# A delta-rule attention with two feed-forward layers on one core: products within a chunk over 128 rows beside the Gram products, and tile 1's matrix handed to GpSimd in the middle of VectorE's first inverse

## The reference

```
k_n = k / (norm(k) + 1e-6)
for t in range(S):
    y[t]  = q[t] @ state
    v_old = k_n[t] @ state
    state = state + beta[t] * outer(k_n[t], v[t] - v_old)
```

## Time and profile before

| | us |
|---|---|
| median of 3 runs | 1130.83 (1129.53 to 1133.27) |
| the profiled execution, its own time | 1131.52 |
| span of the profiled execution | 1129.7 |
| TensorE matmuls busy | 1026.9 |
| VectorE busy | 870.2 |
| ScalarE busy | 779.8 |
| GpSimd busy | 227.1 |

### The profile page before, as it was taken

How to read it: one execution, slowest core, us unless ns; L and a number is a source line. 1 busy time by engine, 2 the same in 40 slices (tenths; PEclk the granted TensorE clock), 3 DMA queues, 4 the chain that set the end, 5 groups by cost and what they waited for, 6 DMA issues and landing times.

```text
span 1129.7 us, 24251 instructions
## 1 busy us (share of the span) xinstructions
PE 1026.9 (91%) x10280; PEld 816.6 (72%) x10280; DVE 870.2 (77%) x948; ACT 779.8 (69%) x991; POOL 227.1 (20%) x380
## 2 busy tenths in 40 slices
PE   4488888888778999999999997999999999999997
PEld 3266666666667888777787876778888888888885
DVE  5966666565388888897887868999787878888885
ACT  1133444465598999989989987986776767676764
POOL 5087888880000010010010000000000000000000
PEclk7578999899989999999999999999999999999999
DMA  7823443323443333435234363430100001010000
GB/s 178 237 60 101 115 130 101 84 77 101 118 91 77 80 91 73 111 63 123 56 67 116 60 168 85 121 112 1 57 1 23 32 0 56 0 56 1 29 1 28
DMA packets 35104, 86.99 MB, mean 77 GB/s; under 512 B 4416, under 2 KB 12096, under 8 KB 35008
## 3 DMA queue, kind: packets, MB, share of 16 engines
q1 hardware_dynamic: 27584, 59.13, 17.3%
q0 software_dynamic: 6912, 25.17, 11.7%
q10 hardware_dynamic: 512, 1.31, 0.5%
HBM read 46.27 MB, written 14.16 MB: 53 GB/s over the span
## 4 chain that ended last, share of the span: by engine, by line
PE 34%; DVE 20%; ACT 12%; issue 6%; DMA 1%; ACTq 0%; DVEq 0%; POOLq 0%
PE o_ps L874 6%; PE o_ps L875 6%; PE o_ps L876 6%; PE h_ps L874 6%; PE h_ps L876 6%; PE h_ps L875 6%; DVE val L1098 5%; DVE den L1055 5%; ACT rec L962 4%; DVE pa L1061 3%; ACT rec L970 2%; DVE val L1082 2%; ACT pa L938 2%; DMA val<-pa 1%; DVE den L1089 1%
## 5 line engine op out<-in xcount | busy, mean ns | idle before, releaser
L874 PE MATMUL o_ps<-g_hi,w_hi_early 128*128 128x512 f32 x288 | 115.6, 401 | 20.8 <-DVE g_lo L1104 15.4
L951 ACT ACTIVATE g_hi<-val 128x1024 fp32r<-128x1024 f32 x96 | 102.0, 1062 | 41.8 <-DVE val L1098 36.1
L865 POOL DMA_DIRECT2D val<-pa x48 | 41.4, 862 | 424.5 <-DVE pa L1061 424.5
L874 PE MATMUL o_ps<-g_hi,w_hi_late 128*128 128x512 f32 x288 | 114.1, 396 | 10.4 <-DVE g_lo L1104 9.9
L1098 DVE SCALAR_TENSOR_TENSOR val<-den,val 128x1024 f32<-128x1024 f32 x96 | 117.4, 1222 | 5.0
L1082 DVE TENSOR_TENSOR val<-val,rec 128x1024 f32<-128x1024 f32 x96 | 117.0, 1219 | 5.5 <-DMA val<-pa 5.5
L1104 DVE SCALAR_TENSOR_TENSOR g_lo<-val,g_hi 128x1024 fp32r<-128x1024 f32 x96 | 117.7, 1226 | 2.0 <-ACT g_hi L951 2.0
L875 PE MATMUL o_ps<-g_lo,w_hi_early 128*128 128x512 f32 x288 | 113.9, 396 | 0.0
L876 PE MATMUL o_ps<-g_hi,w_lo_early 128*128 128x512 f32 x288 | 113.5, 394 | 0.0
L874 PE MATMUL h_ps<-x_hi,w_hi_early 128*128 128x512 f32 x288 | 112.3, 390 | 0.7 <-DVE x_lo L1108 0.4
L875 PE MATMUL o_ps<-g_lo,w_hi_late 128*128 128x512 f32 x288 | 112.9, 392 | 0.0
(11 more groups left out here) (114 smaller groups left out, 2175.4 us busy)
## 6 DMA issues: line engine op xcount, KB each, us to landing
val<-pa POOLq DMA_DIRECT2D x48, 512.0 KB, 4.6
w_raw<-w SPq DMA_DIRECT2D x16, 768.0 KB, 5.1
kv_run<-kv_n SPq DMA_DIRECT2D x24, 384.0 KB, 3.8
x_raw<-x_dram SPq DMA_DIRECT2D x12, 768.0 KB, 5.7
kq<-kq_t SPq DMA_DIRECT2D x44, 192.0 KB, 4.0
x_dram<-stage SPq DMA_DIRECT2D x12, 384.0 KB, 4.3
x_dram<-stage SPq DMA_DIRECT2D x6, 768.0 KB, 4.2
out<-stage SPq DMA_DIRECT2D x5, 768.0 KB, 4.1
```

The costliest lines, as they stand in the source:

```text
L874: nc.tensor.matmul(dst, hi, rhs_hi, start=first, stop=False)
L951: act_fn(g_hi[:, n % 2], val[:, n % 2], ACT.Copy, scale=-1.0).then_inc(g_hi_ready, 1)
```

## The change

1. `wide(tau, c)` holds where both steps of a chunk lie beside Gram products: all chunks of tiles 0, 1, 2 and chunks 0 and 1 of tile 3, 28 steps. There `within` takes 4 products over all 128 rows and columns in place of 16 over 32. For that ScalarE spreads `p_mat` into a block-diagonal `p_blk` (four ACTIVATEs a chunk, one for each batch, two in each step, plus four for the first chunk before the steps), and VectorE makes `u_row`, u without its four copies, right after u_blk. TensorE waits for both before the wide products.
2. VectorE stops its inverse of tile 0 after 16 of 31 rounds, does weights(1), the four scale_gram(1) and turn_n(1), then the other 15 rounds. GpSimd's inverse of tile 1 waits for turn_n(1) only.
3. The buffer k_norm is dropped. The keys for the norms go to x_raw (tiles 0 and 2 to 5) and stage (tile 1). Tile 3's keys are loaded after sums(2), and its sums, roots, root_inverse and weights stand later in tile 0. The first load of x for the feed-forward part comes at the end of tile 3's steps in place of tile 2's.

```diff
+def wide(tau, c):
+    return tau < T and len(gram_parts(tau, G2 * c + 1)) > 0
...
-        k_norm = sb("k_norm", [P, CG, D])
+        u_row = sb("u_row", [P, G2, U, D])
+        p_blk = sb("p_blk", [P, 2, HEADS, B, C])
...
             def load_norm(j):
-                if j >= RING:
-                    sp.wait_ge(sumsq_ready, 1 if j == RING else j)
+                if j >= 2:
+                    sp.wait_ge(sumsq_ready, 1 if j == 2 else j)
...
-            load_norm(3)
...
-                if tau and tau + 3 < T:
+                if tau + 3 < T:
                     load_norm(tau + 3)
...
-                if tau == 2:
+                if tau == 3:
+                    sp.wait_ge(sumsq_ready, T)
...
             def within(tau, c, g):
                 q = index(tau, c, g)
                 pe.wait_ge(q_done, q + 1)
+                if wide(tau, c):
+                    pe.wait_ge(p_ready, CT * tau + c + 1)
+                    pe.wait_ge(urow_ready, q + 1)
                 by_event()
                 for v in range(V):
                     for r in range(HALVES):
+                        at = D * (HALVES * v + r)
+                        if wide(tau, c):
+                            last = nc.tensor.matmul(y_bank[g][:, at:at + D],
+                                                    p_blk[:, c % 2, U * g + V * r + v].rearrange("p b t -> p (b t)"),
+                                                    u_row[:, g, V * r + v],
+                                                    start=False, stop=True, skip_group_check=True)
+                            continue
...
+            def spread_p(tau, c, half):
+                if half == 0:
+                    act.wait_ge(gram_used, 4 * tau + 2 * (c // 2) + 2)
+                    if tau or c >= 2:
+                        act.wait_ge(y_done, index(tau, c, 0) - 2)
+                for b in (2 * half, 2 * half + 1):
+                    last = nc.scalar.activation(p_blk[:, c % 2, :, b], p_mat[:, tau % RING, HEADS * c:HEADS * c + HEADS],
+                                                ACT.Copy, scale=blk_mask[:, b:b + 1])
+                if half:
+                    last.then_inc(p_ready, 1)
...
+                    if c + 1 < CT and wide(tau, c + 1):
+                        spread_p(tau, c + 1, g)
+                    if c + 1 == CT and wide(tau + 1, 0):
+                        spread_p(tau + 1, 0, g)
-                    if s == 1 and tau + 3 < T:
+                    if s == (1 if tau else 3) and tau + 3 < T:
                         squares(tau + 3)
...
             def updates(tau, c, g):
...
+                if wide(tau, c):
+                    dve_tt(u_row[:, g], hz_ps[:, 0:U * D].rearrange("p (u d) -> p u d", u=U),
+                           wgt[:, tau, cg:cg + U].unsqueeze(2).broadcast_to([P, U, D]), ALU.mult).then_inc(urow_ready, 1)
...
-            rounds(dve, dve_tt, 0, 1, dve_step, 0, C - 1, 0)
-            turn_x(0, 0, half_k)
-            turn_x(0, half_k, C)
-            residual(0, 0, 0)
-            spread_w(0)
+            rounds(dve, dve_tt, 0, 1, dve_step, 0, C - 1, C // 2 - 1)
             weights(1)
             for f in range(4):
                 scale_gram(1, f)
             turn_n(1, 0, half_k)
             turn_n(1, half_k, C)
+            rounds(dve, dve_tt, 0, 1, dve_step, C, C // 2 - 1, 0)
+            turn_x(0, 0, half_k)
+            turn_x(0, half_k, C)
+            residual(0, 0, 0)
+            spread_w(0)
...
+                    if (tau, s) == (0, 7):
+                        root_inverse(3)
...
-                    if s == (5 if tau == 0 else 4) and tau + 3 < T:
+                    if tau and s == 4 and tau + 3 < T:
                         root_inverse(tau + 3)
```

More of the change, by code:

```diff
@@ L560, in _ @@
             split = {(T - 2, 1): 0, (T - 2, 5): 1, (T - 1, 1): 2, (T - 1, 5): 3}
+            act.wait_ge(masks_loaded, 32)
+            for half in range(2):
+                spread_p(0, 0, half)
             for tau in range(T):
@@ L630, in scale_gram @@
                 dve.wait_ge(gram_done, 4 * j + f + 1)
+                if r == 0 and j >= RING:
+                    dve.wait_ge(p_ready, CT * (j - RING) + 2 * cp + 2)
                 if f == 0 and j:
@@ L749, in _ @@
                         sums(2, 0, CG)
-                    if fill == 1 and tau + 3 < T:
+                    if s == (1 if tau else 4) and tau + 3 < T:
                         sums(tau + 3, 0, half_n)
-                    if fill == 2 and tau + 3 < T:
+                    if s == (2 if tau else 5) and tau + 3 < T:
                         sums(tau + 3, half_n, CG)
```

11 lines of the change are left out of this document (5 added, 6 removed).

## The result

The changed kernel takes 1146.49 us (median of 5 runs, 1139.16 to 1155.37) against 1131.52 us (1129.53 to 1134.82), a ratio of 1.0139 with a 95% interval of [1.0108, 1.0171]: 15 us slower, where 1123 us was forecast. Its profiled execution is its fastest, 1139.16 us (span 1137.1, granted clock 0.959); the other four show 0.941 to 0.953. So the profile shows about half of the loss; the longer runs are the ones with the lower clock.

A forecast was written before the change was run, and what follows sets the result against it. TensorE was taken to outrun its instruction packets. Ordinary steps -12.2, changeovers +1.6, clock -1.5, helpers +0.5, start +2 and moved root_inverse +1.6 summed to -8.0 us: 1123 us for the median, own range 1118 to 1128 (1111 to 1133 with rivals' far parts).

The forecast's parts named there:

- The price on the array: Wide products on TensorE: eight passes with 128-column weight loads take 0.89 us against 0.36, +0.53 us a step (0 to +1.14).
- A clean wide step: A delta-rule step with wide products: 4.15 us without waits, 4.38 with packets later than the mean, against 4.91 before.
- The first two steps: Tile 0's first two steps, behind the burst: 8.2 us if the clock stays full, against 11.46, so -3.2 us.
- the sum: Terms without the start: ordinary steps -12.2, changeovers +1.6, clock -1.5, VectorE's helper +0.5, moved root_inverse(3) +1.6 us.
- Part 3: The start: tile 0's inverse split, GpSimd beside its last 15 rounds (+0.5 us); net +2 us, between +1.0 and +5.7.
- Part 2: Helpers: ScalarE's p_blk fits in idle time at no cost; VectorE's u_row mostly hidden, +0.5 us in all (0 to 8).
- Part 1: Wide products in 28 steps: 1,344 fewer instructions, 5.4 packets; -12.2 us in 23 ordinary steps, +1.6 in three changeovers.
- the clock, -1.5 us: TensorE's clock in the delta-rule steps: shorter stands give fewer falls, -1.5 us, between 0 and -4.
- Nobody waited for it: GpSimd's inverse of tile 1 ends before 94.31 us, the next tile's burst is at 101.48; an earlier end is worth 0.
- C: Rival: each packet still costs a 0.6 us stand, so added array time isn't absorbed; +15.2 us, 1146 us; chance 0.12.
- B: Rival: u_row and p_blk become waits (+5), the start costs +5; 1131 to 1132 us; chance 0.13 shared with another rival.
- The packets: TensorE's instruction packets, 248 instructions each, come every 4.58 us and hold up the steps; 5.4 fewer with wide products.

The follow-up runs named there:

- gate_ri6: best with split start, GpSimd held until VectorE's last round, tile 3's squares, sums, roots a step earlier and root_inverse(3) in step 6; 1133.10 us, ratio 1.0003 to before.
- early: The changed kernel with keys of tiles 4 and 5 loaded half a tile earlier and ScalarE's squares ahead of p_blk; 1139.82 us, ratio 1.0051 to before.
- best: nosplit and early together: the changed kernel with the start of before and the early squares; 1129.44 us, ratio 0.9965 to before; again on another chip 1134.38 us, 1.0015.
- the narrow kernel: Small products, no p_blk or u_row: best so changed 1138.29 us (1.0025 to before); the changed kernel so changed, split start kept, 1144.40 us (1.0079).
- gate: The changed kernel, with GpSimd beginning tile 1's inverse only after VectorE's last round of its own; 1140.40 us, ratio 1.0074 to before.
- nosplit: The changed kernel with the start of before: VectorE's whole first inverse, then the block for tile 1; 1139.78 us, ratio 1.0041 to before.
- best_pad: best with 24 unread one-column matmuls in each wide step, 48 more instructions; 1144.15 us, ratio 1.0082 to before.
- the first three groups: The follow-up runs from gate to narrow_fill, each group on a chip of its own beside runs of the kernel before; medians 1129.44 to 1144.40 us.
- narrow_fill: best without wide products, p_blk and u_row, plus 6 dummy matmuls in each of 28 Gram steps; 1138.95 us, ratio 1.0044 to before.

## Why the prediction was wrong

**Right.** TensorE stood for its instructions, not for VectorE: issue waits went from 19.3 to 4.9 us with 5 packets fewer. The price on the array was +0.66 us against +0.53, 28 x 0.13 = 3.6 us more in all. A clean wide step took 4.28 us, where 4.15 was said for one without waits, and 4.38 with late packets. The first two steps ran at full clock in 8.2 us, as said. From the third step to tile 3's step 4 the sum had -10.0 (-12.2 + 1.6 - 1.5 + 0.5 + 1.6). The changed kernel's profile has 142.5 us for 141.6 there; without the 13 us of the late squares that is -12.1. gate_ri6 has -6.9. So the saving of the wide products was sound in kind, and of about the size said in one profile, of two thirds of it in another. In that one profile the whole account is: the start +6.2 where +2 was said, the late squares +13 where nothing was, the rest -12.1 where -10.0 was; together +7.1 in place of -8.0.

**Wrong, the largest: Part 3, "With GpSimd running beside the last 15 rounds I add 0.5 us".** Measured +6.1 us on the rounds (17.3 for 11.2). Part 3's net +2 was +8.5 (early less best), or +5.3 for the narrow kernel. With the two inverses apart the first solve comes at 60.06 (gate), where it was forecast. The upper end of its range, +5.7, was no bound: it was made of clock and loads, and the engines' operations side by side had no price from both sides.

**Wrong: Part 2, ScalarE "fits. Nothing, unless it delays the copy of the state half".** It took ScalarE's idle time in a clean step as cover. In step 1 of tiles 1 and 2 the squares stand behind p_blk, and VectorE's sums and u_blk behind the squares. VectorE's stand for them grew from 2.59 to 3.89 us, and with the waits for packets gone it came through to TensorE as twice 2.9 us, with a low clock behind: 13 us in the profile, 7.9 us over the runs (nosplit less best). Even the 2.59 us, which the trace of before shows and of which rows 4 have 1.4, had no place in the sum: Part 1 took the end of the packet waits as the end of all waits. The instruction to look at was not the copy but the one whose reader is queued ahead of u_blk.

**Wrong in its sign: the clock, -1.5 us.** Fewer stands of packets, but longer ones for VectorE; the median granted clock of the changed kernel's runs is 0.952, against 0.958 in the profile of before, and its longer runs are those with the lower clock (0.959 for 1139 us, 0.941 for 1155).

**Left out: "Nobody waited for it" of GpSimd.** True of tile 1's inverse and of before. But the four next ones run without a pause to 255.6 us, 2.2 us ahead of their reader. A forecast of -8 us could hardly have arrived even with everything else as said. Of the rivals, C gave 1146 us, the measured time, by luck: it had each packet costing its stand, and those stands went. B named the right kind, helpers and start turned into waits, with 5 us for each, and gave 1131 to 1132.

**The packets** were a term with the right sign and the wrong law. I had them arrive every 4.58 us; in the trace of before they start 3.3 to 6.0 us apart, and best_pad ran 248 instructions in 3.99 us for three steps without a stand. That pace was what TensorE had used, not a limit. What sets the stands (at 3.2 us of own work for 248 instructions they sum to some 20 us, at 4.0 to 4.6 us to 5 to 9) is left open.

## What to carry to other kernels

An engine that gets new work in front of an old instruction delays whoever reads the old one: follow each instruction behind the insertion to its reader, and see what is queued behind that reader. A wait that another one hides comes out when the other is removed: list the stands of every engine in the trace of before, also those that nobody waited for. Before counting a gain on the bound engine, find the slower chains beside it that run without pause, and read how much room their last link has; a gain beyond that room isn't paid out. Where work is moved so that two element engines run together, price it from a stretch in which they already do, not from each alone.

## What the runs showed of the hardware

VectorE and GpSimd, both on small two-operand operations from SBUF, don't overlap freely: VectorE's 31 elements took 0.69 us beside GpSimd's 252 and 0.19 alone, and the pair advanced in step, at about the pace of the slower (15 rounds in 17.3 us; VectorE takes 11.2 alone, and GpSimd 16.4 behind VectorE's inverse). It goes both ways: the shorter operation is drawn out to the longer, as GpSimd's second operation of 31 elements was beside VectorE's 255.

```profile
44.59 0.41 POOL L223 TENSOR_TENSOR inv<-inv,inv_t 128x31 f32<-128x31 f32 x1
```

It takes 0.25 to 0.27 us in the inverses that run later. The Trainium skill, "SBUF — State Buffer", section "Who interferes with whom", gives VectorE and GpSimd one shared pair of ports, taken for a whole instruction, and names VectorE operations with two SBUF inputs beside a GpSimd operation that reads SBUF. The trace agrees in that the shorter operation ends just behind the longer (60.40 + 0.69 us against 60.36 + 0.67); the two don't simply add up, as the pace stays near GpSimd's own. By this rule +0.5 us for the 15 rounds was too little.

The clock falls in other steps from one execution to the next. In the 13 profiles of the first three groups, of before and of the changed kernel, narrow_fill left out, it fell 66 times between 70 and 280 us, all but once soon after a stand of TensorE of 0.9 us or more (0.85 us that once). Not every stand brings a fall: of 74 stands of 1.4 us or more that began at full clock 55 were followed by one, of 39 between 0.9 and 1.4 us 11. A step wholly at the lower level costs 3.4 us more (7.70 for 4.28 in best). The runs of best lie between 1127.7 and 1145.6 us with a clock of 0.965 to 0.949; twelve runs give a ratio to within 0.3%, and the same kernel on two chips gave 0.9965 and 1.0015. The differences that this case is about are hardly larger.

Instructions have a price of their own on TensorE: 48 more of them in best_pad, 24 matmuls of one column with their weight loads, made a clean step 0.24 us longer, 5 ns each.
